# Attention in a fused kernel: where on TensorE two groups of products and one group of scores stand

## The chip, the cores and the metric

The kernel runs on one core of a Trainium2 chip. The metric is device time in microseconds (us) of one execution, from its start to its end. Three executions of the kernel before gave 857.08, 858.03 and 855.06 us; the median is 857.08 us.

## The reference

Three layers stand one behind the other. The change is in the first.

```python
def _attn_ref(q, k, v):                       # q, k, v: 2 x 8 heads x 1152 x 64, float32
    q_pool = q.reshape(B, H, S // 2, 2, D).mean(axis=3)          # 576 queries
    scores = scale * np.matmul(q_pool, k.transpose(0, 1, 3, 2))  # 576 x 1152
    scores = scores - np.max(scores, axis=-1, keepdims=True)
    attn = np.exp(scores)
    attn = attn / (np.sum(attn, axis=-1, keepdims=True) + 1e-09)
    return np.matmul(attn, v)
...
def reference(**kwargs):
    x = attention rows, 1152 x 512
    x = _moe_ref(x, ...)          # top 2 of 8 experts, 512 -> 1024 -> 512, relu
    return _moe2_ref(x, ...)      # 512 -> 2048, h*cos(h), -> 512
```

## The kernel before, in words

Every engine has its own program, and semaphores tie them together. Attention is the first 310 us or so of the profile; the expert layer and the last layer follow on the same TensorE.

There are 16 heads. Work is staggered: one call of `cycle(p, hh, ...)` (TensorE: L1539, VectorE: L1144, ScalarE: L760) does the attention of one head, prepares the next head, and finishes the head before. The first head's preparation stands ahead of all cycles. So there are 16 cycles: two written out, twelve from a loop of six rounds, and two at the end. The last cycle has no next head to prepare.

A cycle has nine steps, j = 0 to 8, one for each block of 128 keys. In TensorE's order a step can hold:

- **maxima** (`max_scores`, L1454, matmul at L1460): one 128 x 384 piece of raw scores of the next head into PSUM bank 6 or 7. Fifteen pieces make a head, i = 0 to 14. VectorE reduces each one to its row maxima (`max_piece`, L1023). Two banks take turns, so piece i waits (`bank_free`, L1418) until VectorE has reduced piece i - 2. Piece 0 stands in step 0, pieces 1 and 2 in step 1, 3 and 4 in step 2, and so on (`PLACES`, L83).
- **scores of block j** (`scores_t`, L1479, four matmuls at L1490 and L1491): 128 keys x 576 queries of this head, in two parts for precision, into one of two pairs of PSUM banks. Before it starts it waits at L1486 for VectorE to have read the scores of block j - 2, which used the same pair: `at_least(pe, pl_done, s - 1)`.
- **products of block j** (`products`, L1495, six matmuls at L1506 to L1508): the exponentials of block j times v, added up over the nine blocks in banks 4 and 5. It waits for VectorE's low part of block j (`pl_done`). The products of block 0 wait too until ScalarE has copied the sums of the head before out of these banks (`ot_ev`, `o_move`, L747).

Between scores and products a block passes ScalarE twice (L788 writes the rounded exponential `ph`, L793 the exact one in place in PSUM) and VectorE once (`low_p`, L1035: exact less rounded gives `pl`). `ph` and `pl` have three places each, taken in turn: before ScalarE writes `ph` of block j it waits until the products of block j - 3 are done (`av_done`, L786). For block 3 that is the products of block 0.

VectorE's order in a cycle (L1146 to L1156) is written out too: maximum 0; in step 1 maximum 1, `low_p` of block 0, maximum 2; in step 2 maximum 3, `low_p` of block 1, maximum 4; in step 3 maximum 5, `low_p` of block 2, maximum 6; and so on. It is the same in both kernels, and so is ScalarE's.

TensorE's order before, by steps (M = maximum, S = scores, R = products, R' = products of the head before; transposes of step 0 and of step 8 left out):

```
step 0: S0  R'7  M0
step 1: M1  S1   M2  R'8
step 2: M3  S2   M4
step 3: M5  R0   S3  M6  R1
step 4: M7  S4   M8  R2
step 5: M9  S5   M10 R3     (and so on)
```

Of the kernel before, what the change touches and what calls it, by code (L numbers as in the profile page):

```python
# [22 lines left out]
KC = S // P  # L23
# [51 lines left out]
def s_par(hh, j):  # L75

    return (KC * (hh + 1) + j) % 2
# [12 lines left out]
def bank_of(hh, slot):  # L90

    return 6 + (TURNS.index(slot) + hh) % 2
# [11 lines left out]
def present(kind, prep, before, ahead):  # L104

    return {"k": prep, "m": prep, "q": prep, "n": ahead, "o": before}[kind]
# [6 lines left out]
def at_least(eng, sem, value):  # L113

    if isinstance(value, int) and value <= 0:
        return
    eng.wait_ge(sem, value)


def build(nc, q, k, v, w_gate, w_noise, noise, w1, w2, w_in, w_out, out, x_rows, x_slots, y_slots, route):  # L120
    ctx = ExitStack()
    with ctx:
# [145 lines left out]
        def place(name, at, shape, dt=F32):  # L268
            size = 4
            for n in shape[1:]:  # L270
                size *= n
            return nc.alloc_sbuf_tensor_at(name, shape, dt, offset=base + at), -(-(at + size) // 32) * 32
# [115 lines left out]
        hh, at = place("hh", at, [P, FC, P], F32R)  # L388
# [1028 lines left out]
        def _(pe):  # L1417
            def bank_free(p, hh, slot, before, ahead):  # L1418

                n = TURNS.index(slot) - 2  # L1420
                while not present(TURNS[n][0], True, before, ahead):
                    n -= 2
                h = 2 * p + hh - (1 if n < 0 else 0)
                kind, i = TURNS[n]
                if kind == "m":
                    at_least(pe, m_ev, NMAX * (h - 1) + i + 1)
                elif kind == "q":
                    at_least(pe, qb_ev, 2 * h + i + 1)
                    if i == 1:
                        at_least(pe, kq_ev, 4 * (h + 1) + 3)  # L1430
                elif kind == "o":
                    at_least(pe, o_norm, h - 1)
                elif kind == "n":
                    at_least(pe, kq_ev, 4 * (h + 1) + i + 1)
                else:
                    at_least(pe, kq_ev, 4 * h + i + 1)

            def kq_group(p, hh, slot, at, first=False):

                h, par = 2 * p + hh, hh % 2  # L1440
                kind, i = slot
                if i == 0 and not first:
                    pe.wait_ge(kq_ready, h + 1)
                bank = ps[:, at, :]
                if i == 2:
                    pe.transpose(bank[:, P:2 * P], ks[:, par, KC - 1, :, :].rearrange("p t d -> p (t d)"), ident[:, :])
                    last = pe.transpose(bank[:, 2 * P:3 * P], qa[:, QC - 1, :, :].rearrange("p t d -> p (t d)"), ident[:, :])
                else:
                    for a in range(4):
                        src = qa[:, a, :, :] if i == 3 else ks[:, par, i * 4 + a, :, :]  # L1450
                        last = pe.transpose(bank[:, a * P:(a + 1) * P], src.rearrange("p t d -> p (t d)"), ident[:, :])
                last.then_inc(kq_done, 1)

            def max_scores(p, hh, i):  # L1454

                h, par = 2 * p + hh, hh % 2
                if i == 0:
                    pe.wait_ge(kq_ev, 4 * (h + 1))
                a, c = divmod(i, QC)
                pe.matmul(ps[:, bank_of(hh, ("m", i)), 0:PIECE], qat[:, par, c * P:(c + 1) * P],  # L1460
                          kt[:, par, a * PIECE:(a + 1) * PIECE], start=True, stop=True).then_inc(m_done, 1)
# [17 lines left out]
            def scores_t(p, hh, j):  # L1479

                h, par, sp_ = 2 * p + hh - 1, (hh - 1) % 2, s_par(hh, j)
                s = KC * h + j
                if j == 0:
                    pe.wait_ge(k1_done, h + 1)
                    pe.wait_ge(qb_ev, 2 * (h + 1))
                at_least(pe, pl_done, s - 1)  # L1486
                keys = slice(j * P, (j + 1) * P)
                for a in range(2):
                    cols = slice(a * HQ, (a + 1) * HQ)
                    pe.matmul(ps[:, 2 * sp_ + a, 0:HQ], kt[:, par, keys], qat[:, par, cols], start=True, stop=False)  # L1490
                    last = pe.matmul(ps[:, 2 * sp_ + a, 0:HQ], k1[:, par, keys], qbt[:, par, cols],  # L1491
                                     start=False, stop=True)
                last.then_inc(st_done, 1)

            def products(p, hh, j):  # L1495

                h, par = 2 * p + hh - 1, (hh - 1) % 2
                s = KC * h + j
                pe.wait_ge(pl_done, s + 1)
                if j == 0:  # L1500
                    pe.wait_ge(v_ready, h + 1)
                    at_least(pe, ot_ev, h)
                for a in range(2):
                    cols = slice(a * HQ, (a + 1) * HQ)
                    dst = ps[0:D + 1, 4 + a, 0:HQ]
                    pe.matmul(dst, vs[:, par, j, 0, :], ph[:, j % 3, cols], start=(j == 0), stop=False)  # L1506
                    pe.matmul(dst, vs[:, par, j, 0, :], pl_[:, j % 3, cols], start=False, stop=False)  # L1507
                    last = pe.matmul(dst, vs[:, par, j, 1, :], ph[:, j % 3, cols], start=False, stop=(j == KC - 1))  # L1508
                last.then_inc(av_done, 1)

            def rank_of(b, bank):

                cols = slice(b * QC, (b + 1) * QC)
                pe.wait_ge(scan_done, b + 1)
                pe.matmul(ranks_at(bank), tri[:, :], member[:, :, cols], start=True, stop=False)
                last = pe.matmul(ranks_at(bank), ones[:, :], upto[:, :, cols], start=False, stop=True)
                last.then_inc(rank_done, 1)
                if b == 1:
                    pe.matmul(ps[:, COUNTS, 0:E], ones[:, :], upto[:, :, RT - 1], start=True, stop=True
                              ).then_inc(rank_done, 1)  # L1520
# [18 lines left out]
            def cycle(p, hh, main, prep, before, av_before, ahead=True, early=False):  # L1539
                for j in range(KC):  # L1540
                    if early and j == 0:
                        scores_t(p, hh, 0)
                    if j == 7 and not prep:
                        pe.wait_ge(o_norm, NHEAD - 2)
                        pe.wait_ge(qb_ev, 2 * NHEAD)
                        rank_of(0, RANK0)
                    for n, slot in enumerate(PLACES[j]):
                        if slot and present(slot[0], prep, before, ahead):
                            kind, i = slot
                            if prep:  # L1550
                                bank_free(p, hh, slot, before, ahead)
                            else:
                                pe.wait_ge(qb_ev, 2 * NHEAD)
                            if kind == "k":
                                kq_group(p, hh, slot, bank_of(hh, slot))
                            elif kind == "n":
                                kq_group(p, hh + 1, slot, bank_of(hh, slot))
                            elif kind == "m":
                                max_scores(p, hh, i)
                            elif kind == "q":  # L1560
                                if i == 1 and ahead:
                                    kq_group(p, hh + 1, TAIL, bank_of(hh, slot))
                                qb_group(p, hh, i)
                            else:
                                turn_o(p, hh - 2)
                        if n == 0 and main and not (early and j == 0):
                            if j == 3:
                                products(p, hh, 0)
                            scores_t(p, hh, j)
                        if n == 1:  # L1570
                            if j > 2 and main:
                                products(p, hh, j - 2)
                            elif j < 2 and av_before:
                                products(p, hh - 1, j + KC - 2)

            pe.wait_ge(consts_done, 4)
            for i in range(WARM):
# [25 lines left out]
            pe.wait_ge(k1_filled, 2)  # L1603
            pe.wait_ge(gate_in, 64)
            cycle(0, 1, True, True, False, False, early=True)
            cycle(0, 2, True, True, True, True, early=True)
            with pe.Fori(1, NHEAD // 2 - 1) as p:
# [202 lines left out]
```

## Time and profile before

| what | value |
|---|---|
| median of three runs | 857.08 us (855.06 to 858.03) |
| profiled execution, its own time | 854.54 us |
| span of the profile, first to last instruction | 852.8 us |
| TensorE matmuls busy | 838.9 us, 98% of the span |
| VectorE busy | 499.0 us, 59% |
| ScalarE busy | 422.2 us, 50% |
| GpSimd busy | 402.5 us, 47% |
| share of DMA queue q1 of 16 engines' time | 23.5% |

The profile is of one execution. Busy TensorE time counts a matmul until its modelled end, and neighbours overlap, so a busy share of 98% doesn't show every gap: gaps are read as the distance between the starts of two matmuls. The median of the runs is 2.5 us above the profiled execution.

### The profile page before, as it was taken

What the parts mean: (1) busy time and instruction counts of PE and PEld (TensorE: products, weight loads), DVE (VectorE), ACT (ScalarE), POOL (GpSimd) and SP (SyncE); (2) the same over time, 40 slices, a digit from 0 to 9 for tenths busy, and PEclk for the clock granted to TensorE, in tenths of its full rate; (3) what the DMA queues carried; (4) which work ended last, traced back from release to release, by engine and by line L of the source; (5) the groups of instructions that cost most, each with busy time, mean ns of one, the idle gap of its engine ahead of it and who ended that gap; (6) DMA issues with size and microseconds to landing.
All of it is one profiled execution on the core that took longest, in us unless ns stands there. A gap on an engine that the chain in (4) does not pass through costs nothing.

```text
span 852.8 us, 15404 instructions
## 1 busy us (share of the span) xinstructions
PE 838.9 (98%) x4868; PEld 744.4 (87%) x4869; DVE 499.0 (59%) x995; ACT 422.2 (50%) x776; POOL 402.5 (47%) x293
## 2 busy tenths in 40 slices
PE   7999999999999999999999999999999999999998
PEld 6899999999999888888887888888888888999997
DVE  7788877888877887322232222222276776676664
ACT  3777777777777763212111211111145665564554
POOL 8554445555877104648959959577532030000000
PEclk9999999999999999999999999999999999999999
DMA  5112211142232015987645545363444020000101
GB/s 146 53 43 62 64 42 42 42 142 67 92 130 102 1 56 181 310 298 241 237 151 172 197 148 184 118 214 115 155 133 152 1 75 27 12 1 0 38 1 38
DMA packets 51521, 91.28 MB, mean 107 GB/s; under 512 B 9376, under 2 KB 18592, under 8 KB 50976
## 3 DMA queue, kind: packets, MB, share of 16 engines
q1 hardware_dynamic: 40832, 67.26, 23.5%
q0 software_dynamic: 3360, 11.01, 4.4%
q10 hardware_dynamic: 7296, 12.59, 4.4%
q8 instruction: 19, 0.31, 0.2%
q14 instruction: 14, 0.11, 0.0%
HBM read 73.78 MB, written 17.06 MB: 107 GB/s over the span
## 4 chain that ended last, share of the span: by engine, by line
PE 89%; DVE 5%; ACT 2%; issue 2%; POOL 2%; DMA 0%; DVEq 0%; POOLq 0%; ACTq 0%
PE ps L1640 10%; PE ps L1642 10%; PE ps L1641 10%; PE ps L1460 5%; PE ps L1490 5%; PE ps L1506 4%; PE ps L1508 4%; PE ps L1507 4%; PE ps L1491 4%; PE ps L1766 4%; PE ps L1767 4%; PE ps L1765 4%; PE ps L1752 3%; PE ps L1750 3%; PE ps L1751 3%; PE ps L1679 2%
## 5 line engine op out<-in xcount | busy, mean ns | idle before, releaser
L639 POOL TENSOR_TENSOR W<-stage,W 128x2048 fp32r<-128x2048 f32 x32 | 147.3, 4602 | 2.6
L1023 DVE TENSOR_REDUCE mx<-ps 128x1 f32<-128x384 f32 x225 | 119.6, 551 | 17.8 <-PE ps L1460 17.8
L1035 DVE TENSOR_TENSOR pl__80<-ps,ph 128x576 fp32r<-128x576 f32 x144 | 108.0, 750 | 33.5 <-ACT ps L793 33.4
L788 ACT ACTIVATE ph<-ps 128x576 fp32r<-128x576 f32 x144 | 93.9, 652 | 53.5 <-PE ps L1491 52.4
L793 ACT ACTIVATE ps<-ps 128x576 f32<-128x576 f32 x144 | 93.5, 649 | 0.0
L1506 PE MATMUL ps<-ph,vs 128*65 128x288 f32 x288 | 86.1, 299 | 0.4 <-ACT ot L747 0.4
L862 ACT CAST hh<-ps 128x512 fp32r<-128x512 f32 x50 | 26.9, 590 | 119.2 <-PE ps L1679 115.2
L1490 PE MATMUL ps<-qat,kt 128*128 128x288 f32 x288 | 83.8, 306 | 1.3 <-ACT qbt L740 0.6
L1508 PE MATMUL ps<-ph,vs 128*65 128x288 f32 x288 | 84.8, 294 | 0.0
L1507 PE MATMUL ps<-pl__80,vs 128*65 128x288 f32 x288 | 84.6, 294 | 0.0
L1640 PE MATMUL ps<-W,xh 128*128 (+1 forms) x200 | 80.4, 402 | 1.3 <-POOL W L639 0.7
L1640 PE MATMUL ps<-W,hh 128*128 (+1 forms) x200 | 80.4, 402 | 0.0
L1491 PE MATMUL ps<-qbt,k 128*128 128x288 f32 x288 | 80.3, 294 | 0.0
L1642 PE MATMUL ps<-W,xl 128*128 (+1 forms) x200 | 78.3, 392 | 0.0
L1642 PE MATMUL ps<-W,hl 128*128 (+1 forms) x200 | 78.3, 391 | 0.0
L1641 PE MATMUL ps<-W,hh 128*128 (+1 forms) x200 | 77.9, 390 | 0.0
L1641 PE MATMUL ps<-W,xh 128*128 (+1 forms) x200 | 77.8, 389 | 0.0
L1460 PE MATMUL ps<-kt,qat 128*128 128x384 f32 x225 | 76.2, 352 | 1.6 <-ACT qat L727 0.9
L1300 DVE COPY ys<-ps 128x512 f32<-128x512 f32 x25 | 17.3, 691 | 96.5 <-PE ps L1642 96.5
L1288 DVE TENSOR_SCALAR hid<-ps 128x512 f32<-128x512 f32 x25 | 17.3, 692 | 91.9 <-PE ps L1642 87.7
L1750 PE MATMUL ps<-fh,W 128*128 128x384 f32 x192 | 64.9, 338 | 0.0
L1752 PE MATMUL ps<-fh,W 128*128 128x384 f32 x192 | 64.8, 337 | 0.0
(220 smaller groups left out, 1960.8 us busy)
## 6 DMA issues: line engine op xcount, KB each, us to landing
stage<-in_moe_w_dram SPq DMA_DIRECT2D x32, 1024.0 KB
y_slots<-ys ACTq DMA_DIRECT2D x25, 256.0 KB
x_slots<-ring SPq DMA_DIRECT2D x22, 256.0 KB
xs<-x_slots ACTq DMA_DIRECT2D x22, 256.0 KB
kn<-in_k_dram SPq DMA_DIRECT2D x16, 288.0 KB, 3.3
vn<-in_v_dram SPq DMA_DIRECT2D x16, 288.0 KB, 2.8
stage<-in_moe_w_in_dram SPq DMA_DIRECT2D x4, 1024.0 KB
stage<-in_moe_w_out_dram SPq DMA_DIRECT2D x4, 1024.0 KB
```

What stands on the lines that cost most here:

```text
L639: pl.tensor_tensor(W[:, slot, 1, part], stage[:, j % 2, :], W[:, slot, 0, part].bitcast(F32), ALU.subtract).then_inc(w_ready, 1)
L1023: ve.tensor_reduce(mx3[:, i:i + 1], ps[:, bank_of(hh, ("m", i)), 0:PIECE], AX_X, ALU.max).then_inc(m_ev, 1)
L1035: ve.tensor_tensor(pl_[:, j % 3, :].rearrange("p (a n) -> p a n", a=2), ps[:, 2 * s_par(hh, j):2 * s_par(hh, j) + 2, 0:HQ], ph[:, j % 3, : ...
L1460: pe.matmul(ps[:, bank_of(hh, ("m", i)), 0:PIECE], qat[:, par, c * P:(c + 1) * P], kt[:, par, a * PIECE:(a + 1) * PIECE], start=True, stop ...
L1490: pe.matmul(ps[:, 2 * sp_ + a, 0:HQ], kt[:, par, keys], qat[:, par, cols], start=True, stop=False)
L1491: last = pe.matmul(ps[:, 2 * sp_ + a, 0:HQ], k1[:, par, keys], qbt[:, par, cols], start=False, stop=True)
L1506: pe.matmul(dst, vs[:, par, j, 0, :], ph[:, j % 3, cols], start=(j == 0), stop=False)
L1507: pe.matmul(dst, vs[:, par, j, 0, :], pl_[:, j % 3, cols], start=False, stop=False)
L1508: last = pe.matmul(dst, vs[:, par, j, 1, :], ph[:, j % 3, cols], start=False, stop=(j == KC - 1))
L1640: pe.matmul(dst, hi, rhs_of(i, 0), start=(i == 0), stop=False)
L1641: pe.matmul(dst, hi, rhs_of(i, 1), start=False, stop=False)
L1642: last = pe.matmul(dst, lo, rhs_of(i, 0), start=False, stop=(i == n - 1))
```

## The change

Only the order of TensorE's instructions in a cycle changes; none is added, removed or resized, and the waits stay with the groups that they belong to. The products of block 8 of the head before (R'8) stand ahead of maximum 2 instead of behind it, in the fourteen cycles that have both. The scores of block 3 (S3) stand ahead of the products of block 0 (R0) instead of behind them, in all sixteen.

```
step 0: S0  R'7  M0
step 1: M1  S1   R'8 M2
step 2: M3  S2   M4
step 3: M5  S3   R0  M6  R1
step 4: M7  S4   M8  R2
```

```diff
                         if n == 0 and main and not (early and j == 0):
+                            scores_t(p, hh, j)
                             if j == 3:
                                 products(p, hh, 0)
-                            scores_t(p, hh, j)
+                        if n == 0 and j == 1 and av_before:
+                            products(p, hh - 1, KC - 1)
                         if n == 1:
                             if j > 2 and main:
                                 products(p, hh, j - 2)
-                            elif j < 2 and av_before:
-                                products(p, hh - 1, j + KC - 2)
+                            elif j == 0 and av_before:
+                                products(p, hh - 1, KC - 2)
```

## Rows read from the trace of the kernel before

**Rows 1.** Page, part 1: engine, busy us, share of the span, instructions.

```profile
PE 838.9 (98%) x4868; PEld 744.4 (87%) x4869; DVE 499.0 (59%) x995; ACT 422.2 (50%) x776; POOL 402.5 (47%) x293
```

**Rows 2.** Page, part 4: the chain that ended last, by engine.

```profile
PE 89%; DVE 5%; ACT 2%; issue 2%; POOL 2%; DMA 0%; DVEq 0%; POOLq 0%; ACTq 0%
```

**Rows 3.** Waits, 20 to 310 us: who <- for whom: us in total, times, longest.

```profile
PEld ps L1460 <- DVE mx L1023: 7.8, 31, 0.5
PEld ps L1490 <- DVE pl__80 L1035: 1.8, 6, 0.5
```

**Rows 4.** Timeline, TensorE, one cycle: start us, us, engine, line, operation, count.

```profile
111.64 0.29 PE L1491 MATMUL ps<-qbt,k 128*128 128x288 f32 x1
111.96 0.44 PE L1460 MATMUL ps<-kt,qat 128*128 128x384 f32 x1
112.24 0.29 PE L1506 MATMUL ps<-ph,vs 128*65 128x288 f32 x1
...
113.20 0.30 PE L1490 MATMUL ps<-qat,kt 128*128 128x288 f32 x1
113.33 0.29 PE L1491 MATMUL ps<-qbt,k 128*128 128x288 f32 x1
...
113.73 0.74 PE L1460 MATMUL ps<-kt,qat 128*128 128x384 f32 x2
114.31 0.29 PE L1506 MATMUL ps<-ph,vs 128*65 128x288 f32 x1
...
115.10 0.29 PE L1490 MATMUL ps<-qat,kt 128*128 128x288 f32 x1
...
115.64 0.34 PE L1460 MATMUL ps<-kt,qat 128*128 128x384 f32 x1
...
116.61 0.34 PE L1460 MATMUL ps<-kt,qat 128*128 128x384 f32 x1
...
118.45 0.29 PE L1490 MATMUL ps<-qat,kt 128*128 128x288 f32 x1
```

**Rows 5.** Timeline, VectorE, the same cycle.

```profile
111.35 1.02 DVE L1023 TENSOR_REDUCE mx<-ps 128x1 f32<-128x384 f32 x2 [0.69 <-PE ps L1460]
112.29 0.75 DVE L1035 TENSOR_TENSOR pl__80<-ps,ph 128x576 fp32r<-128x576 f32 x1
112.95 1.01 DVE L1023 TENSOR_REDUCE mx<-ps 128x1 f32<-128x384 f32 x2
113.88 0.75 DVE L1035 TENSOR_TENSOR pl__80<-ps,ph 128x576 fp32r<-128x576 f32 x1
...
116.98 0.56 DVE L1023 TENSOR_REDUCE mx<-ps 128x1 f32<-128x384 f32 x1 [0.29 <-PE ps L1460]
117.45 0.75 DVE L1035 TENSOR_TENSOR pl__80<-ps,ph 128x576 fp32r<-128x576 f32 x1
```

**Rows 6.** Timeline, the last cycle: scores that wait for VectorE, weight load included.

```profile
298.45 0.76 DVE L1035 TENSOR_TENSOR pl__80<-ps,ph 128x576 fp32r<-128x576 f32 x1 [0.43 <-ACT ps L793]
...
299.26 0.19 PEld L1490 LDWEIGHTS ps<-qat,kt 128*128 128x128 f32 x1 [0.33 <-DVE pl__80 L1035]
299.26 0.40 PE L1490 MATMUL ps<-qat,kt 128*128 128x288 f32 x1
...
299.50 0.29 PE L1491 MATMUL ps<-qbt,k 128*128 128x288 f32 x1
```

**Rows 7.** Timeline, the cycle before the last: low part of block 1, products of block 0.

```profile
278.46 0.75 DVE L1035 TENSOR_TENSOR pl__80<-ps,ph 128x576 fp32r<-128x576 f32 x1
...
278.88 0.29 PE L1506 MATMUL ps<-ph,vs 128*65 128x288 f32 x1
```

**Rows 8.** Timeline, the last cycle: low part of block 1, products of block 0.

```profile
295.30 0.76 DVE L1035 TENSOR_TENSOR pl__80<-ps,ph 128x576 fp32r<-128x576 f32 x1
...
295.60 0.32 PE L1506 MATMUL ps<-ph,vs 128*65 128x288 f32 x1 [0.37 <-ACT ot L747]
```

**Rows 9.** Timeline, ScalarE, the cycle of rows 4: rounded exponential of block 3.

```profile
115.84 0.66 ACT L788 ACTIVATE ph<-ps 128x576 fp32r<-128x576 f32 x1 [0.71 <-PE ps L1491]
```

## The prediction

> **What bounds the kernel now.** I read the page's busy shares first: TensorE is at 98%, no other engine above 59% [rows 1]. The chain that ended last says the same, 89% of it TensorE, 5% VectorE [rows 2]. So a change of order on TensorE can give or cost only what it does to TensorE's gaps. Next come the waits within attention: the weight load of a maximum (L1460) waited 31 times for VectorE's reduction of a piece two places back, 7.8 us in all, and scores (L1490) waited 6 times for VectorE's low part, 1.8 us [rows 3]. That is all of VectorE's that TensorE waits for in 290 us. The timeline of one cycle from the loop then shows where the gaps lie and what VectorE does meanwhile; a gap is the distance of two starts less the usual distance. The usual distances: six products take 115.10 - 114.31 = 0.79 us, 0.13 each; a score matmul 113.33 - 113.20 = 0.13; four of them and the next maximum start 115.64 - 115.10 = 0.54 apart; between maxima 6 (115.64) and 7 (116.61) lie 0.97 us, less 0.79 for the products 0.17 to 0.18 for the maximum; I use 0.17 [rows 4].
>
> There are two gaps in the cycle. (a) At maximum 2: 111.64 to 111.96 is 0.32 where 0.13 is usual, and the next start comes 0.28 later where 0.17 is usual, so 0.19 + 0.11 = 0.30 us are lost. (b) At maximum 5: maxima 4 and 5 start at 113.73 and the following product at 114.31, 0.58 where 2 x 0.17 is usual, so 0.24 us [rows 4]. Behind 114.31 I see no other gap: from maximum 7 at 116.61 to S5 at 118.45 are 1.84 us, and M7, S4, M8, R2 and M9 make 3 x 0.17 + 0.53 + 0.79 = 1.83 [rows 4].
>
> VectorE's side is what decides. From 111.35 its starts follow each other closely: two maxima, low part 0 (ends 112.29 + 0.75 = 113.04), maxima 2 and 3 (end 112.95 + 1.01 = 113.96), low part 1 (ends 113.88 + 0.75 = 114.63) [rows 5]. It has no idle time in this stretch, so these ends are set by when maxima 0 and 1 arrive and by VectorE alone, not by TensorE's order between 111.4 and 114.6.
>
> **The change part by part.**
>
> *Products of the head before ahead of maximum 2.* R'8 waits for nothing new: its low part was done in the previous cycle. It starts at 111.64 + 0.13 = 111.77, takes 0.79, and maximum 2 starts at 112.56, long after the reduction of maximum 0 ended (111.35 + half of 1.02 and a little more, about 111.91). So gap (a) goes, 0.30 us. What is late next is S2. It must wait for low part 0, which ends at 113.04. The wait's own delay and its restart I take from scores that waited for the same producer: low part ends 298.45 + 0.76 = 299.21, the load and the matmul start at 299.26, 0.05 later, and the second matmul 0.24 after the first instead of 0.13, so 0.11 of restart [rows 6]. TensorE would be free for S2 at 112.56 + 2 x 0.17 = 112.90; it starts at 113.09, and its second matmul at 113.33. Before, the second matmul stood at 113.33 as well [rows 4]. The gap has moved from M2 to S2, and this part is worth nothing: 0.00, with bounds of -0.11 (if the restart is not paid) and +0.06.
>
> The +0.06 is for VectorE: maximum 2 arrives later now. From maximum 7, a piece that VectorE waited for, start to reduction is 116.98 - 116.61 = 0.37 [rows 4, 5]. Maximum 2 then arrives at 112.56 + 0.37 = 112.93, VectorE wants it at 112.95 [rows 5]: just in time in the loop. In the second cycle and the one before the last, the same walk misses by 0.06 (I worked it through each cycle's own starts). I take 0.06 in two cycles, 0 in the twelve of the loop; the upper bound is 0.06 in all fourteen, 0.8 us. ScalarE's copy of the sums (L747) may start once R'8 is done; ScalarE does it after its exponential of block 1, which has not moved, so that gains nothing.
>
> *Scores of block 3 ahead of the products of block 0.* M4 and M5 stand as before: M5 waits for the reduction of maximum 3, which ends at 113.96, and what follows it can start at 114.31. Before, that was R0, ready to go, and its 0.79 us covered the last 0.37 us until S3's condition was met: S3 waits for low part 1, which ends at 114.63. Now S3 comes first and nothing covers the wait. All that queues behind it on TensorE waits too: R0, M6, R1 and the rest of the cycle. S3 starts at 114.63 + 0.05 = 114.68, and with 0.11 of restart the stream runs as if from 114.79. The same work (S3, R0, then M6) used to start at 114.31. The cost is 114.79 - 114.31 = 0.48 us in a cycle. The cycle before the last gives 278.46 + 0.75 + 0.05 + 0.11 - 278.88 = 0.49 [rows 7], and the same difference lies between 0.48 and 0.50 in all fifteen cycles with maxima.
>
> Is it given back later in the cycle? No gap is left behind R0 that could take it up. Does it grow? S3's earlier start does not bring the exponential forward: ScalarE's `ph` of block 3 needs the products of block 0 done, and these now stand behind S3. It started at 115.84, right behind S3 [rows 9]; now it follows R0, at about the old start of M6 plus 0.48 less 0.13 plus 0.29 plus 0.05, so 116.33, again 0.49 later. Its exact twin ends some 1.2 us after that, 117.5, before VectorE takes low part 3 at 117.45 + 0.48 = 117.93 [rows 5]. S5 is the one to watch: low part 3 would end at 117.93 + 0.75 = 118.68, S5 would come at 118.45 + 0.48 = 118.93, so the margin of 0.25 us stays [rows 4, 5].
>
> The last cycle has no maxima. R0 stood at 295.60, itself held by ScalarE's copy; low part 1 ended at 296.06 [rows 8]. S3 effectively at 296.06 + 0.16 = 296.22 costs 0.62; less 0.03 of R0's own restart, 0.59. Later waits for low parts (as in rows 6) move with it, because `ph` of block 3 hangs on R0 here too. I take 0.55, with bounds 0.3 and 0.65.
>
> **A rule weighed.** A load that waits starts together with its matmul, at 299.26 [rows 6]: it was not done ahead, and that is the 0.11 of restart. The Trainium skill ("TensorE: Matmul & The Clock Gate", section "Architectural detail: the array is 16× 32×32, not 1× 128×128") says that TensorE's queue can pull a weight load ahead of matmuls in flight. If that held across a wait for a semaphore, the restart would be hidden and the sum would be 16 x 0.11 = 1.8 us less. The row speaks against it, since the wait stands before the load.
>
> **Sum.** 15 x 0.48 = 7.2; + 2 x 0.06 = 0.1; + 0.55 for the last cycle: 7.9 us slower. Behind attention nothing absorbs it: the expert layer starts from attention's rows, and TensorE is the chain there too [rows 2]. Profiled execution: 854.54 + 7.9 = 862.4 us. The median before lies 2.5 us above that execution, so for the median 857.08 + 7.9 = 865.0 us.
>
> **Rivals.**
>
> 1. *The waits are met on arrival (the other side, faster).* If low part 0 and low part 1 were ready when TensorE came, gap (a) would go for good and S3 before R0 would be free: 14 x 0.30 = 4.2 us, 852.9 us. For it: gap (a) is real and R'8 does fill it. Against: it decides at S2 and S3, and for that low part 0 would have to end by 112.85 and low part 1 by 114.26, where the rows have 113.04 and 114.63. VectorE would have to be 0.2 to 0.4 us ahead with the same work.
> 2. *The delay is given back.* If the cycle's later part had slack that only looks like work, for instance if TensorE's tail of a cycle were held by something else than its own stream, S3's wait costs nothing: within 1 us of 857. Against: no gap behind 114.31 [rows 4] and a 98% busy TensorE [rows 1].
> 3. *The restart is hidden.* 15 x 0.37 + 0.44 = 6.0 us: 863.1 us. Against: rows 6.
> 4. *The delay grows.* The margin of 0.25 us at S5 is eaten up, since VectorE's maxima now stand 0.48 later against low parts that stayed. Each 0.1 us beyond it costs 0.1 in each of 15 cycles; with 0.06 of late VectorE everywhere and 0.14 at S5 it is 15 x 0.20 = 3.0 us more, 868.0 us. Against: both ends of the margin move by the same 0.48.
>
> **How the numbers follow.** Forecast 70%, restart hidden 7%, delay grows 10%, given back 7%, met on arrival 6%. What a measurement of this kernel can tell from no change is about 0.3%, 2.6 us. The first three are slower by more than that: 0.87. Given back is within it: 0.07. Met on arrival is faster: 0.06. The forecast's own bounds: 15 x 0.37 to 15 x 0.54, with 0.3 to 0.65, is 5.9 to 8.8, so 863.0 to 865.9. The three runs before spread over 3 us, so the median of a kernel is uncertain by about 1 on either side: 862.0 to 866.9. Stretched toward rival 4: 861.8 to 867.6; that leaves out rivals 1 and 2 and the far end of 4.
>
> **What the changed profile would show.** Right: maximum 2 no longer has a wait ahead of it; S2 (L1490) waits for low part 0 some 0.2 us in each cycle and S3 some 0.4 us for low part 1, so the row of L1490 waiting for L1035 grows from 6 waits to over 30 and the row of L1460 waiting for L1023 falls to about half its count, M5's gap being left. A cycle of the loop is 0.5 us longer. VectorE's starts up to low part 1 are unchanged against maximum 0. Wrong: S3 follows M5 at about 0.28 us, as R0 did, with no wait; or S2 starts without a wait behind M3; or a cycle of the loop keeps its old length although S3 waits; or a new wait stands at S5.

## The result and the profile after

The changed kernel takes 862.28 us in the median of five runs (861.84 to 863.35), the kernel before 856.00 us in the median of its five (853.78 to 858.03). The ratio is 1.0077, with a 95% interval of 1.0055 to 1.0099: 6.6 us slower, between 4.7 and 8.5. The forecast was 865.0 us and a growth of 7.9; the two profiled executions, 854.54 and 862.28 us, lie 7.7 apart.

The page of the kernel after: the span, the busy shares (to be held against [rows 1]) and the chain by engine (against [rows 2]).

```profile
span 860.6 us, 15404 instructions
...
PE 843.2 (98%) x4868; PEld 745.2 (87%) x4869; DVE 501.5 (58%) x995; ACT 421.2 (49%) x776; POOL 401.6 (47%) x293
...
PE 84%; DVE 9%; ACT 2%; issue 2%; POOL 2%; DMA 0%; DVEq 0%; POOLq 0%; ACTq 0%
```

Busy time has hardly moved, and the instructions are the same in number. What has moved is the chain: TensorE's share fell from 89% to 84% and VectorE's rose from 5% to 9%, since the chain now runs through VectorE wherever scores wait for a low part.

The waits of the kernel after from 20 to 318 us, the same view as [rows 3]: who waited for whom, us in total, times, longest. A wait stands under the weight load (PEld) or the matmul (PE) of a line, so the two rows of L1490 belong together.

```profile
ACT ph L788 <- PE ps L1508: 20.7, 16, 1.7
PEld ps L1490 <- DVE pl__80 L1035: 14.5, 35, 1.1
...
PE ps L1490 <- DVE pl__80 L1035: 4.4, 17, 0.9
PEld ps L1460 <- DVE mx L1023: 4.4, 17, 0.6
```

Maxima waiting for VectorE fell from 31 times to 17: 15 of these are M5, so the gap at M2 is gone from fourteen cycles and that at M5 is left. Scores waiting for a low part rose from 6 weight loads to 35: S2 and S3 of all sixteen cycles and three more. The first row is new: sixteen times, once a cycle, ScalarE waited for products (L1508) before it could write `ph`. That is block 3's exponential, which now hangs on the products of block 0.

TensorE's timeline in the same cycle as [rows 4], which begins here 2.74 us later (its first scores at 112.23 instead of 109.49).

```profile
114.39 0.30 PE L1491 MATMUL ps<-qbt,k 128*128 128x288 f32 x1
114.52 0.30 PE L1506 MATMUL ps<-ph,vs 128*65 128x288 f32 x1
...
115.32 0.51 PE L1460 MATMUL ps<-kt,qat 128*128 128x384 f32 x2
115.84 0.40 PE L1490 MATMUL ps<-qat,kt 128*128 128x288 f32 x1
116.08 0.30 PE L1491 MATMUL ps<-qbt,k 128*128 128x288 f32 x1
...
116.49 0.72 PE L1460 MATMUL ps<-kt,qat 128*128 128x384 f32 x2
117.44 0.40 PE L1490 MATMUL ps<-qat,kt 128*128 128x288 f32 x1 [0.23 <-DVE pl__80 L1035]
117.67 0.30 PE L1491 MATMUL ps<-qbt,k 128*128 128x288 f32 x1
...
118.07 0.29 PE L1506 MATMUL ps<-ph,vs 128*65 128x288 f32 x1
```

The weight load of S3, from the timeline of the loads:

```profile
117.43 0.19 PEld L1490 LDWEIGHTS ps<-qat,kt 128*128 128x128 f32 x1 [0.48 <-DVE pl__80 L1035]
```

VectorE's timeline beside it (against [rows 5]).

```profile
114.10 1.02 DVE L1023 TENSOR_REDUCE mx<-ps 128x1 f32<-128x384 f32 x2 [0.70 <-PE ps L1460]
115.04 0.75 DVE L1035 TENSOR_TENSOR pl__80<-ps,ph 128x576 fp32r<-128x576 f32 x1
115.71 1.01 DVE L1023 TENSOR_REDUCE mx<-ps 128x1 f32<-128x384 f32 x2
116.64 0.75 DVE L1035 TENSOR_TENSOR pl__80<-ps,ph 128x576 fp32r<-128x576 f32 x1
```

R'8 (114.52) now fills the old gap at M2: M2 starts right behind it at 115.32, and M3 follows M2 without a wait. But S2 stands at 115.84 where 115.32 + 0.34 = 115.66 was possible, and its second matmul at 116.08. Taken from VectorE's first reduction that is 116.08 - 114.10 = 1.98 us; before it was 113.33 - 111.35 = 1.98 [rows 4, 5]. The gap has changed its place and nothing else. VectorE's own starts, counted from the first, are 0.94, 1.61 and 2.54; before they were 0.94, 1.60 and 2.53. Then comes S3: low part 1 ends at 117.39, S3 starts at 117.44, its second matmul 0.24 later, and R0 (118.07) stands 3.97 us behind VectorE's first reduction instead of 2.96.

### The profile page after: what moved, and what is told of

It reads as the page before. It is cut to its first block, busy times and chain, and to the rows that moved or that the text cites. A ratio compares the mean times of both kernels' runs of the same rounds, so it can differ in the third digit from the quotient of the medians.

```text
span 860.6 us, 15404 instructions
## 1 busy us (share of the span) xinstructions
PE 843.2 (98%) x4868; PEld 745.2 (87%) x4869; DVE 501.5 (58%) x995; ACT 421.2 (49%) x776; POOL 401.6 (47%) x293
## 4 chain that ended last, share of the span: by engine, by line
PE 84%; DVE 9%; ACT 2%; issue 2%; POOL 2%; DMA 0%; DVEq 0%; POOLq 0%; ACTq 0%
PE ps L1642 10%; PE ps L1644 10%; PE ps L1643 10%; PE ps L1490 4%; PE ps L1508 4%; PE ps L1506 4%; PE ps L1507 4%; PE ps L1768 3%; PE ps L1769 3%; PE ps L1767 3%; PE ps L1491 3%; PE ps L1754 3%; PE ps L1752 3%; PE ps L1753 3%; PE ps L1460 3%; DVE mx L1023 3%
## 5 line engine op out<-in xcount | busy, mean ns | idle before, releaser
L1490 PE MATMUL ps<-qat,kt 128*128 128x288 f32 x288 | 86.9, 317 | 5.9 <-DVE pl__80 L1035 4.4
L1506 PE MATMUL ps<-ph,vs 128*65 128x288 f32 x288 | 86.1, 299 | 0.0
L1508 PE MATMUL ps<-ph,vs 128*65 128x288 f32 x288 | 84.9, 295 | 0.0
L1460 PE MATMUL ps<-kt,qat 128*128 128x384 f32 x225 | 72.7, 346 | 1.3 <-ACT qat L727 0.9
L1490 PEld LDWEIGHTS ps<-qat,kt 128*128 128x128 f32 x288 | 54.2, 188 | 16.2 <-DVE pl__80 L1035 14.5
L1752 PE MATMUL ps<-fh,W 128*128 128x384 f32 x192 | 65.0, 339 | 0.0
```

## The experiments

Each was timed in five rounds beside the kernel before, which had 855.67 us (29 runs) in the first set and 855.63 us (23 runs) in the second. Because the executions of one kernel spread over some 4 us, I also give "attention": from the first matmul of scores to the start of the last matmul at L1506 (the products' line), in the profiled execution. It is 289.94 us before and 297.78 after, 7.84 apart. And a "cycle": the distance of the first scores of two cycles, mean over eleven of the loop. It is 18.27 us before and 18.75 after.

**1. The first part alone.** S3 stays behind R0.

```diff
+                        if n == 0 and j == 1 and av_before:
+                            products(p, hh - 1, KC - 1)
                         if n == 1:
...
-                            elif j < 2 and av_before:
-                                products(p, hh - 1, j + KC - 2)
+                            elif j == 0 and av_before:
+                                products(p, hh - 1, KC - 2)
```

> Only the first part: products of the head before (R'8) ahead of maximum 2; scores of block 3 stay behind the products of block 0. My theory: VectorE's chain sets when the scores of block 2 may start, so the wait moves from M2 to S2 and the time stays: 0 us, between -1.5 and +0.8. The wait of L1460 for L1023 falls from 31 times to some 17, the wait of L1490 for L1035 rises by some 14. Rival (the gap at M2 was worth its size): 14 x 0.30 = 4.2 us faster.

Measured: 855.76 us, ratio 0.9995 (0.9981 to 1.0009); attention 290.05, cycle 18.26. The waits of this kernel:

```profile
PEld ps L1490 <- DVE pl__80 L1035: 6.4, 20, 0.5
PEld ps L1460 <- DVE mx L1023: 4.4, 17, 0.6
```

Fourteen waits left the maxima and fourteen came to the scores, and the time is the same. The rival of 4.2 us is out. The 0.06 us that I had put down for a late VectorE shows where I had placed it: the second cycle and the one before the last are each 0.08 us longer than before (18.90 against 18.82, 17.78 against 17.70). In passing: this profiled execution has a span of 854.7 us, 1.9 above the one before, though attention is the same to 0.1 us. Its first scores start at 19.81 us instead of 17.68: part of the spread between executions lies ahead of the first cycle.

**2. The second part alone.** R'8 stays behind M2.

```diff
+                            scores_t(p, hh, j)
                             if j == 3:
                                 products(p, hh, 0)
-                            scores_t(p, hh, j)
```

> Only the second part: scores of block 3 ahead of the products of block 0; R'8 stays behind M2. My theory: the whole cost of the change, 0.48 us in each of 15 cycles and 0.5 in the last, 7.8 us slower than before, the same as the full change within 0.8 us. Rival (the two parts cost together, through VectorE getting maximum 2 later): about half of it, 4 us.

Measured: 863.71 us, ratio 1.0090 (1.0070 to 1.0111), 7.7 us slower; attention 297.66, cycle 18.75. Its waits:

```profile
PEld ps L1490 <- DVE pl__80 L1035: 9.9, 21, 1.1
PEld ps L1460 <- DVE mx L1023: 7.8, 31, 0.5
PE ps L1490 <- DVE pl__80 L1035: 4.4, 17, 0.9
```

The maxima wait 31 times as before, and the whole cost is there. So this part is the cause, and the two parts don't cost together.

**3. The other way round: R0 one place up, ahead of M5.** The rest is the kernel before.

```diff
                     for n, slot in enumerate(PLACES[j]):
+                        if j == 3 and n == 0 and main:
+                            products(p, hh, 0)
                         if slot and present(slot[0], prep, before, ahead):
...
-                            if j == 3:
-                                products(p, hh, 0)
                             scores_t(p, hh, j)
```

> The opposite of the second part: from the kernel before, the products of block 0 go one place up, ahead of maximum 5 (order M3 S2 M4 R0 M5 S3 M6 R1). My theory: gap (b), 0.24 us at M5, is filled by R0, which waits only for ScalarE's copy (ends 113.86, R0 comes at 113.90), and S3 then comes at 114.87, behind the end of low part 1 (114.63). 0.24 us less in 14 cycles of the loop's kind: 3.3 us faster than before; 1.8 us if R0 just misses the copy and pays a restart of 0.11 each time. Rival (VectorE, getting M5 0.05 us late, or the copy takes the gap's place): no change.

Measured: 853.89 us, ratio 0.9978 (0.9965 to 0.9991), 1.9 us faster, between 0.8 and 3.0; attention 288.88, 1.06 less; cycle 18.21. The medians meet the lower one of my two figures (1.8), but in the profiled executions only 1.06 us lie in attention, the only part where the order differs. Its timeline, TensorE, from M4 on:

```profile
113.57 0.33 PE L1460 MATMUL ps<-kt,qat 128*128 128x384 f32 x1
113.85 0.32 PE L1506 MATMUL ps<-ph,vs 128*65 128x288 f32 x1
114.00 0.30 PE L1507 MATMUL ps<-pl__80,vs 128*65 128x288 f32 x1
...
114.66 0.34 PE L1460 MATMUL ps<-kt,qat 128*128 128x384 f32 x1
114.84 0.29 PE L1490 MATMUL ps<-qat,kt 128*128 128x288 f32 x1
```

M5 (114.66) and S3 (114.84) now follow without a gap: R0 covers VectorE's time, as said. But R0 comes 0.28 us behind M4 where 0.17 is usual. ScalarE's copy, which it waits for:

```profile
113.07 0.64 ACT L747 COPY ot<-ps 65x576 f32<-65x576 f32 x1
```

It ends at 113.71, R0 starts 0.14 later. I had allowed 0.05, so R0 "just misses the copy", but not as I had priced it. The restart is small: 0.15 us from R0 to its second product where 0.13 is usual, not 0.11 more. The delay is the larger part, and it differs: the cycle shown has 0.28 us from M4 to R0 and gains about 0.10 us; in every second cycle of the loop it is 0.35, and the gain is 0.01 to 0.05. So most of what M5's gap gives is lost there.

**4. R0 ahead of M5, and R'8 ahead of M2 as in the change** (the edits of 3 and 1 together).

> Both: products of block 0 ahead of maximum 5 and R'8 ahead of maximum 2. My theory holds the place of R'8 to be worth nothing, so this is the run with the products of block 0 alone moved up, within 0.8 us: about 3 us faster than before. Rival (R'8's place counts once M5's gap is gone): 4 us or more apart from that run.

Measured: 852.91 us, ratio 0.9971 (0.9959 to 0.9983), 2.5 us faster than before; attention 287.69, cycle 18.11. Its timeline, M2 and M3, S2, then M4, R0, M5 and S3:

```profile
111.64 0.51 PE L1460 MATMUL ps<-kt,qat 128*128 128x384 f32 x2
112.19 0.40 PE L1490 MATMUL ps<-qat,kt 128*128 128x288 f32 x1
112.42 0.30 PE L1491 MATMUL ps<-qbt,k 128*128 128x288 f32 x1
...
112.83 0.33 PE L1460 MATMUL ps<-kt,qat 128*128 128x384 f32 x1
113.03 0.32 PE L1506 MATMUL ps<-ph,vs 128*65 128x288 f32 x1
...
113.85 0.34 PE L1460 MATMUL ps<-kt,qat 128*128 128x384 f32 x1
114.03 0.29 PE L1490 MATMUL ps<-qat,kt 128*128 128x288 f32 x1
```

By the medians this run and experiment 3 are 1.0 us apart, which their intervals do not separate; by attention they are 1.2 us apart. I had expected less than 0.8, so that is a small miss. The places explain it: with R'8 earlier the sums are ready earlier, and ScalarE copies them earlier. In experiment 3 the copy (113.07) started 0.04 us after R'8's last product had ended, so it hung on R'8; here it starts 0.45 us after that end, behind ScalarE's own exponentials. R0 stands 0.20 us behind M4 instead of 0.28 in this cycle and of 0.35 in every second one, and the mean cycle is 0.10 us shorter. So R'8's place, worth nothing as long as S2 and M5 wait for VectorE, gets a small worth, 1.2 us, once R0 waits for the copy. This kernel is faster than both kernels of the case.

**5. The change with less work for VectorE.** Maxima 2 and 3 are reduced over 64 of their 384 columns, in the order of the change and in that of before. These two pieces leave columns out of the row maxima.

```diff
-                ve.tensor_reduce(mx3[:, i:i + 1], ps[:, bank_of(hh, ("m", i)), 0:PIECE], AX_X, ALU.max).then_inc(m_ev, 1)
+                ve.tensor_reduce(mx3[:, i:i + 1], ps[:, bank_of(hh, ("m", i)), 0:PIECE if i not in (2, 3) else 64], AX_X,
+                                 ALU.max).then_inc(m_ev, 1)
```

> The changed kernel, with VectorE's reductions of maxima 2 and 3 cut from 384 to 64 columns in every cycle (so these two pieces leave columns out of the row maxima). VectorE then comes to low part 1 some 0.6 us earlier. My theory: the wait of the scores of block 3 and that of M5 shrink to nothing or nearly, the order as such costs nothing, and the time is 1 to 3.4 us under the kernel before, within 2.8 us of the same cut in the order of before. Rival (the order costs by itself, for instance because ScalarE's exponential of block 3 now hangs on the products of block 0): it stays 6 to 8 us above the same cut in the order of before.

> The kernel before with the same cut of VectorE's maxima 2 and 3 to 64 columns, to be read against the run above. My theory: only the gap at M5 goes, 0.24 us in 14 or 15 cycles: 3.4 us faster than before.

Measured: with the change's order 854.49 us, ratio 0.9991 (0.9980 to 1.0003), attention 288.64, cycle 18.14; with the order of before 851.58 us, ratio 0.9958 (0.9942 to 0.9974), attention 286.30, cycle 18.05. The latter is 3.6 us less than before in attention and 4.1 by the medians, where I had expected 3.4. In the loop the order now costs 0.09 us a cycle instead of 0.48. The timeline of the change's order with shorter maxima (the line numbers are one higher), VectorE and TensorE:

```profile
112.94 0.36 DVE L1023 TENSOR_REDUCE mx<-ps 128x1 f32<-128x64 f32 x2
113.25 0.76 DVE L1036 TENSOR_TENSOR pl__80<-ps,ph 128x576 fp32r<-128x576 f32 x1
```

```profile
113.71 0.51 PE L1461 MATMUL ps<-kt,qat 128*128 128x384 f32 x2
114.06 0.40 PE L1491 MATMUL ps<-qat,kt 128*128 128x288 f32 x1
114.30 0.30 PE L1492 MATMUL ps<-qbt,k 128*128 128x288 f32 x1
```

Low part 1 ends at 114.01, S3 starts at 114.06, at its usual distance behind M4 and M5 (0.35), and still shows the restart (0.24 to the next start). That is the 0.1 us left. The total stays 2.3 us apart in attention, inside my 2.8, and 2.9 by the medians, just above it; the rival, 6 to 8 us, is out. Of the 2.3, 0.65 lies in the last cycle, which has no maxima and so nothing that was shortened (16.68 against 16.03 us), 0.31 in the cycle before it, and the rest mostly the restarts. ScalarE's exponential of block 3 hangs on the products of block 0 in this order too, so that link costs nothing in the loop.

**6. Maximum 0 ahead of the last of R'7's matmuls,** on top of experiment 4, to start VectorE's chain earlier.

```diff
                     pe.matmul(dst, vs[:, par, j, 0, :], pl_[:, j % 3, cols], start=False, stop=False)
+                    if a == 1 and ahead_of_last:
+                        ahead_of_last()
                     last = pe.matmul(dst, vs[:, par, j, 1, :], ph[:, j % 3, cols], start=False, stop=(j == KC - 1))
...
+                                def first_maximum():
+                                    bank_free(p, hh, ("m", 0), before, ahead)
+                                    max_scores(p, hh, 0)
+                                products(p, hh - 1, KC - 2, first_maximum if prep else None)
```

> The products of block 0 ahead of M5 and R'8 ahead of M2, and besides, maximum 0 stands ahead of the last one of R'7's six matmuls: VectorE's chain of the cycle, which sets when S2 may start, begins 0.13 us earlier. My theory: S2's remaining wait (0.20 us and the restart) shrinks by 0.13 in each of 14 cycles: 1.8 us faster than without that, some 4.5 us faster than before. Rival (bank 6 is not free yet, since VectorE still reads the turned output of the head before, or VectorE's idle time before M0 has another cause): same as without, or slower by a new wait of up to 0.2 us a cycle.

Measured: 854.46 us, ratio 0.9991 (0.9981 to 1.0001); attention 288.85, 1.2 us more than experiment 4; cycle 18.19. TensorE's weight load and matmul of M0:

```profile
110.64 0.19 PEld L1460 LDWEIGHTS ps<-kt,qat 128*128 128x128 f32 x1 [0.16 <-issue]
110.65 0.44 PE L1460 MATMUL ps<-kt,qat 128*128 128x384 f32 x1
110.92 0.30 PE L1510 MATMUL ps<-ph,vs 128*65 128x288 f32 x1
```

and VectorE beside it:

```profile
110.28 0.23 DVE L1062 TENSOR_TENSOR shares<-ps,rinv 128x80 f32 x1
111.21 0.56 DVE L1023 TENSOR_REDUCE mx<-ps 128x1 f32<-128x384 f32 x1 [0.70 <-PE ps L1460]
```

The rival holds in this cycle. M0's bank holds the turned output of the head before, which VectorE reads until 110.51. M0 starts only behind that, pays a restart, and VectorE's idle time before its first reduction is 0.70 us, as it was in the kernel before, 0.69 [rows 5]. In every second cycle of the loop that idle time is longer in experiment 4, 0.78 us, and there it does fall, to 0.70, so VectorE's chain begins 0.08 us earlier. That wins nothing either, because R0 now waits for ScalarE's copy. M0's wait and restart push the scores of block 1 back, the exponential of block 1 waits for them, and the copy stands behind it. VectorE's first reduction and ScalarE's exponential of block 1 in experiment 4:

```profile
110.44 1.02 DVE L1023 TENSOR_REDUCE mx<-ps 128x1 f32<-128x384 f32 x2 [0.70 <-PE ps L1460]
111.13 0.65 ACT L788 ACTIVATE ph<-ps 128x576 fp32r<-128x576 f32 x1 [0.48 <-PE ps L1491]
```

and here that exponential, the copy and R0:

```profile
112.03 0.65 ACT L788 ACTIVATE ph<-ps 128x576 fp32r<-128x576 f32 x1 [0.61 <-PE ps L1491]
...
113.15 0.64 ACT L747 COPY ot<-ps 65x576 f32<-65x576 f32 x1
...
113.93 0.32 PE L1506 MATMUL ps<-ph,vs 128*65 128x288 f32 x1
```

R0 stands 113.93 - 111.21 = 2.72 us behind VectorE's first reduction, in experiment 4 113.03 - 110.44 = 2.59: 0.13 us more, as much as ScalarE's wait has grown.

## Why the prediction was right, point by point

- *The first part is worth nothing.* Right, by experiment 1: 0.1 us of attention, 0.00 in a cycle of the loop. The reason holds too: S2 is set by low part 0, and S2's second matmul stands 1.98 us behind VectorE's first reduction in both kernels. One sentence on the way there was not right: that R'8's place does not move ScalarE's copy of the sums. In the kernel before the copy (113.22) started 0.04 us after R'8's last product had ended, so it did hang on R'8; but R0 came 0.44 us behind the copy's end there, and in the changed kernel it stands behind S3, so nothing hung on it.
- *VectorE gets maximum 2 just in time.* Right in the loop: its starts up to low part 1 shift by 0.01 us. In the second cycle and the one before the last I had 0.06 us each; experiment 1 shows 0.08.
- *The second part costs 0.48 in a cycle.* Right: 18.75 - 18.27 = 0.48, and experiment 2 shows that it is this part alone.
- *Delay 0.05 and restart 0.11 for scores that wait.* Right: 117.39 to 117.44, and 0.24 to the next start.
- *The `ph` of block 3 moves behind R0 without cost in the loop.* Right: sixteen new waits of ScalarE for products, and no new wait at S5 in the loop, where the scores still come 0.25 us behind the end of low part 3, the margin that I had worked out; experiment 5 keeps this link and drops to 0.1 us a cycle.
- *Nothing is given back.* Nearly. In the cycle before the last I had 0.54 us, and it is 18.04 - 17.70 = 0.34. There VectorE has extra reductions, and S5, S6 and S7 waited for low parts before the change. The delay swallowed S5's wait with its restart (0.12 us) and shortened what stands ahead of S6 (0.09 us). I had looked for slack only in the loop.
- *The last cycle.* I had 0.55, measured 0.69 (16.73 against 16.04). The two misses, -0.20 and +0.14, nearly cancel: that the sum agrees to 0.1 us is in part luck.
- *The sum.* 7.9 forecast, 7.84 in attention. The level, 865.0, is 2.7 us above the measured median: I had added the 2.5 us by which the median of three runs of before lay above its profiled execution, and with more runs that difference is 1.5 (856.00) and 1.1 us (855.67). The growth of the medians, 6.3 us, is inside the interval of the ratio together with 7.8. That interval, 4.7 to 8.5 us, also holds the 6.0 us of rival 3, so the times alone do not rule the hidden restart out; the trace does.
- *A rule weighed.* By the Trainium skill ("TensorE: Matmul & The Clock Gate", section "Architectural detail: the array is 16× 32×32, not 1× 128×128"), a weight load can be pulled ahead of matmuls in flight. At S3 load (117.43) and matmul (117.44) start together behind the wait, and 0.24 us pass to the next start; the rule does not reach across a wait for a semaphore here, and the 6.0 us of that rival are too low against the 7.84 us of attention.

## What to carry to other kernels

When two engines each do a part of the same chain, first find which of them sets the next start, here VectorE from its first reduction to low part 1, and leave ready work on the other one in front of the instruction that waits for it. Work moved into one gap is worth nothing if the next instruction waits for the same chain; and work taken out from in front of a wait costs as much as it had covered, plus the restart. Moving a group also moves what other engines do with its result: R'8 set when ScalarE could copy, and M0 when the scores of block 1 came. To find the better order, list for each wait when it can be met at the earliest, and put the groups whose conditions are met first: that gave the 0.3% of experiment 4.

## What the runs showed of the hardware that I had not expected

Not every wait ends 0.05 us after its condition. From the end of ScalarE's copy to the start of the products that wait for it are 0.14 us in experiment 3, and from the end of VectorE's last reading of the bank (110.51) to M0 in experiment 6 also 0.14, while scores that wait for a low part start 0.05 us behind it. M5 starts 0.06 us behind the reduction that it waits for (113.96 to 114.02 in the kernel before). It is not the loop with its computed wait values: in the last cycle, which stands outside it, the copy ended at 295.46 us and the products started at 295.60, 0.14 again.

```profile
294.82 0.64 ACT L747 COPY ot<-ps 65x576 f32<-65x576 f32 x1
...
295.60 0.32 PE L1506 MATMUL ps<-ph,vs 128*65 128x288 f32 x1 [0.37 <-ACT ot L747]
295.76 0.30 PE L1507 MATMUL ps<-pl__80,vs 128*65 128x288 f32 x1
```

These groups have several waits one behind the other, the scores of blocks 1 to 8 and M5 only one; whether that makes the difference was not tried. At these places a wait that is "just met" is not met.

The restart is not the same for every group either. For scores and maxima the next start comes 0.10 to 0.11 us later than usual (S3 0.24, M0 in experiment 6 0.27). For the products of block 0 it comes only 0.02 to 0.03 later (0.15 in experiment 3, 0.16 above). Why was not tried.
